# Moving the first sums of squares into the last attention pair, in an attention + gated MLP + routed experts kernel

## The chip, the cores and the metric

The kernel runs on one core of one Trainium2 chip. The metric is device time in microseconds (us) of one execution. Engines: PE is TensorE, ACT is ScalarE, DVE is VectorE, POOL is GpSimd, SP issues most DMAs.

## The reference

All in float32. Three blocks follow each other.

```python
# 1: attention, B=2, H=8, S=768, D=64; the mask keeps pairs whose 6 sign bits q@proj, k@proj agree
scores = where(mask, scale * q @ k.T, -1e9)
attn = exp(scores - max); attn /= attn.sum + 1e-9
x = (attn @ v), heads side by side          # (1536, 512)
# 2: RMS norm and gated MLP, d_ff 1536
xn = x / sqrt(mean(x * x) + 1e-6) * rms_g
y = (silu(xn @ w_gate) * (xn @ w_val)) @ w_out
# 3: one of 8 experts for each token, by argmax of y @ router
out = gate * sigmoid(...) * (relu(y @ w1[e]) @ w2[e])
```

## The kernel before

Each fp32 product is made of rounded "high" parts and remainders ("low" parts), in three matmuls (high x high, high x low, low x high), so that each operand needs a high pass (on ACT) and a low pass (on DVE or POOL).

**Attention** works on 8 pairs of heads, P = 0 to 7, the last with batch 1. One pair has 12 steps j (two heads, six tiles of 128 queries). In a step every engine's `period` does one piece of each stage, in the order of its code, and the stages lag: `scores` of step j on PE (L858, L859) into `ps_s`, `maxes` on DVE (L1441), `exps` on ACT (L1191), normalizing on POOL (L693, once in three steps), then five steps later `turn` on PE (transposes, L872, into `ps_t`), `highs` on ACT (L1201, `pT_h`), `lows` on DVE (L1459, `pT_l`), and six steps later `values` on PE (L887, L889) into a value bank, `ps_o` for even groups g of three steps and `ps_p` for odd ones. When a group's values are complete ACT copies one half (`half_out`, L1206) and DVE adds the other into `xT` (`x_out`, L1465), which counts `x_done` up by one and frees the bank. In full pairs DVE does that at the end of its step, behind its `lows`, seven steps after the group's last score. `period(7, 1, ahead=False)` is the last pair; `period(8, 0, s=False, ahead=False)` is the drain: six steps without scores in which what is left of the pair is turned and multiplied.

**The RMS norm** needs the sum of x*x over 512 columns. Tokens are in four groups tg of 384 (0 and 1 are batch 0, 2 and 3 batch 1). POOL squares and adds (`add_squares`, L652, L656) into two tiles `sums` for each of groups 0 and 1 and one tile for each of groups 2 and 3. PE adds over the partitions with matmuls that stream one column of ones (`sum_squares`, L905), three for each tile, and for groups 2 and 3 three more each for `last_square`, the squares of the last pair, which ACT makes (L1212). They land in the columns of `sum_places`, all in `ps_p`. ACT takes the root (`root`, L1218, with a table load the first time), DVE inverts (`invert`, L1472), PE turns the factors (`turn_rinv`, L930), DVE copies them out (`rows_of_factors`, L1476), and SP spreads them through DRAM. Groups 0 and 1 are summed at step 1 of the drain, behind a wait for `x_done` 30; groups 2 and 3 after it.

**The gated MLP** needs the high parts of xT times the gain (`high_xn`, L1223, on ACT), and low parts: POOL for group 0 (`lows_first`, L667 and L670), DVE for the rest (`lows_xn`, L1481). In the last pair ACT makes the four high parts of batch 0, 768 columns each, at steps 1, 2, 4 and 5. In the drain PE slips in the first products of the MLP (`early_units`, `unit`, L920), by the table `EARLY`: 2, 6, 2, 2, 2 and 2 chunks of three matmuls at steps 0 to 5. After the drain it runs the gate of group 2, whose last chunk waits for the last but one of DVE's `lows_xn`, sums groups 2 and 3, and goes on with its value, the inverse, and group 3. POOL meanwhile squares batch 1 and then splits the next weights (`split_w`, L710 and L713), the second of them as soon as `x_done` is 32. From there PE runs dense MLP work for groups and filters, and later the projection, routing and experts.

Each engine runs its own program in order; semaphores named above tie them.

Of the kernel before, what the change touches and what calls it, by code (L numbers as in the profile page):

```python
# [13 lines left out]
ALU = mybir.AluOpType  # L14
# [18 lines left out]
def build(nc, q, k, v, proj, w_gate, w_val, w_out, rms_g, router, out_gate, w1, w2, out):  # L33
# [6 lines left out]
    HT = T // 2  # L40
# [37 lines left out]
    with ExitStack() as ctx:  # L78
# [179 lines left out]
        for i in range(3):  # L258
# [17 lines left out]
                 "half_ready x_done pool_passed sp_passed "  # L276
                 "consts_made gates_in filled fill_done square_step last_squared summed rms_made rinv_made rinv_turned factors_row factors_out "
                 "gained u_made xnh_made xnl_pool xnl_dve w_split wo_split gate_made value_made sig_made silu_step hs_high hs_low y_made x2_made "
# [8 lines left out]
         half_ready, x_done, pool_passed, sp_passed,  # L287
         consts_made, gates_in, filled, fill_done, square_step, last_squared, summed, rms_made, rinv_made, rinv_turned, factors_row, factors_out,
         gained, u_made, xnh_made, xnl_pool, xnl_dve, w_split, wo_split, gate_made, value_made, sig_made, silu_step, hs_high, hs_low, y_made, x2_made,
# [21 lines left out]
        def cols_of(tg):  # L311
            return slice((tg % 2) * G, (tg % 2 + 1) * G)
# [72 lines left out]
        value_banks = (ps_o, ps_p)  # L385
        sum_places = tuple(ps_p[:, HT * tg:HT * (tg + 1)] for tg in range(TG))

# [3 lines left out]
        def high_of(tg, c):  # L391

            if tg < TG // 2:
                return c + 1
            return C + c + 1 if c < C - 1 else C + c + tg - 1

        XNH_DONE = 2 * C + 1

# [411 lines left out]
        def _(pe):  # L810
# [84 lines left out]
            def sum_squares(tg):  # L895

                pe.wait_ge(square_step, squares_until[tg])
                parts = list(sums[tg])
                if tg >= TG // 2:
                    pe.wait_ge(factors_row, 1)  # L900
                    pe.wait_ge(last_squared, tg - TG // 2 + 1)
                    parts.append(last_square[tg - TG // 2])
                for t in range(HT):
                    for n, part in enumerate(parts):
                        mm = nc.tensor.matmul(sum_places[tg][:, t:t + 1], part[:, t * P128:(t + 1) * P128],  # L905
                                              ones_f[:, 0:1], start=(n == 0), stop=(n == len(parts) - 1))
                mm.then_inc(summed, 1)
# [40 lines left out]
            def period(P, par, before=True, s=True, ahead=True):  # L948
                for j in range(PAIR_STEPS):
                    if s:  # L950
                        scores(P, par, j)
                    if not s and j == 1:
                        pe.wait_ge(x_done, 4 * LAST_PAIR + 2)
                        sum_squares(0)
                        sum_squares(1)
                    if not s and j == 3:
# [7 lines left out]
                    if not s and j in EARLY:  # L964
                        some(EARLY[j], first_units)
                    if not s and j == 2:
                        turn_rinv(0)
# [192 lines left out]
        def _(act):  # L1160
# [54 lines left out]
            def root(tgs):  # L1215
                act.wait_ge(summed, tgs[-1] + 1)
                cols = slice(HT * tgs[0], HT * (tgs[-1] + 1))
                nc.scalar.activation(rms[:, cols], ps_p[:, cols], ACT.Sqrt, bias=eps[:],  # L1218
                                     scale=1.0 / DM).then_inc(rms_made, len(tgs))

            def high_xn(b, c, cols=slice(0, S)):

                nc.scalar.activation(xn[:, b, 0, c, cols], xT[:, C * b + c, cols], ACT.Copy,  # L1223
                                     scale=gain[:, c:c + 1]).then_inc(xnh_made, 1)
# [7 lines left out]
            def period(P, par, before=True, s=True, ahead=True):  # L1232
                for j in range(PAIR_STEPS):
# [6 lines left out]
                    if jj == 2 and ((j >= LAG + 1 and s) or (j < LAG + 1 and before)):  # L1240
                        half_out(Pv, g)
                    if s and not ahead and j in (1, 2, 4, 5):
                        if j == 1:
                            act.wait_ge(gates_in, 48)
                            act.wait_ge(scores_ready, PAIR_STEPS * LAST_PAIR)
                        high_xn(0, (1, 2, 4, 5).index(j))
                    if not s and j in (0, 2, 3):
                        high_xn(1, (0, 2, 3).index(j))
                    if not s and j == 1:
                        root((0, 1))  # L1250
# [161 lines left out]
        def _(dve):  # L1412
# [55 lines left out]
            def invert(tgs):  # L1468
# [3 lines left out]
                nc.vector.reciprocal(rinv[:, cols], rms[:, cols]).then_inc(rinv_made, len(tgs))  # L1472

            def rows_of_factors(b):
                dve.wait_ge(rinv_turned, b + 1)
                nc.vector.tensor_copy(rinv_rows[b][:], ps_p[0:2 * HT, P128:2 * P128]).then_inc(factors_row, 1)  # L1476
# [7 lines left out]
            def period(P, par, before=True, s=True, ahead=True):  # L1484
                for j in range(PAIR_STEPS):
# [4 lines left out]
                    if j == 0 and before:  # L1490
                        denoms(P - 1, 3)
                    if not s and j == 2:
                        invert((0, 1))
# [15 lines left out]
                    if jj == 2 and j < LAG + 1 and not s:  # L1509
                        x_out(Pv, g)  # L1510
                    if not s and j == 2:
                        rows_of_factors(0)
                    if isinstance(P, int) and P == 0 and j in (1, 2, 3, 4):
                        bits_first(1, j - 1)
# [65 lines left out]
            period(8, 0, s=False, ahead=False)  # L1580

            lows_xn(DVE_LOWS[10:12])
            invert((2, 3))
# [242 lines left out]
```

## Time and profile before

| | |
|---|---|
| time, median of 3 runs | 809.3 us (808.05 to 812.13) |
| the profiled execution's own time | 808.94 us |
| its span | 807.2 us |
| PE busy | 766.6 us, 95% of the span |
| DVE, ACT, POOL busy | 62%, 46%, 39% |
| last pair of attention, first scores to the drain's first transposes | 210.0 to 240.0 us |
| drain and first MLP products, to the second filter | 240.0 to 279.3 us |

All times inside the span are from its start. A busy share is an average over very different stages, and TensorE's busy time does not tell at which clock it ran. The chain of waits says who ended last at each moment; the timeline of one engine names, in brackets, how long it sat idle before an instruction and who released it. An fp32 matmul or transpose appears as two records.

### The profile page before, as it was taken

The page shows a single profiled execution, that of the slowest core. Times are in us where ns is not written, and L with a number is a line of the kernel's source. Part 1 is how long each engine was busy: PE and PEld are TensorE (multiplying, and loading weights), DVE is VectorE, ACT ScalarE, POOL GpSimd, SP SyncE. Part 2 cuts the span into 40 slices and gives each one's busy share as a digit, 9 for nine tenths or more (in the row PEclk, how much of TensorE's full clock was granted, in tenths as well). Part 3 has the DMA queues.
Part 4 walks back from the last instruction along what each step waited for, and adds up shares of the span by engine and source line. Part 5 has one row for each costly group of instructions (what it writes and reads, how often), then busy time and mean ns, then how long its engine had stood idle before and what let it go on. Part 6 is the DMA issues. An engine that isn't in the chain of part 4 may idle for free.

```text
span 807.2 us, 14150 instructions
## 1 busy us (share of the span) xinstructions
PE 766.6 (95%) x4212; PEld 677.9 (84%) x4212; DVE 501.6 (62%) x979; ACT 374.7 (46%) x668; POOL 317.8 (39%) x340
## 2 busy tenths in 40 slices
PE   4899999999999999999999999999769999999996
PEld 3799888988878999999999988888548887888784
DVE  7999999999984553443343444363664566555641
ACT  5888888888983311111111234434423335553331
POOL 7877777788886363234422002211200111010110
PEclk9999999999997999999999999999979999999999
DMA  6888769656300321111210030040543365555410
GB/s 197 230 239 223 199 171 271 185 146 149 83 2 27 92 70 61 40 39 39 65 52 0 3 153 27 27 139 29 186 157 131 136 240 204 181 196 196 141 50 22
DMA packets 53716, 96.82 MB, mean 120 GB/s; under 512 B 6841, under 2 KB 21189, under 8 KB 53656
## 3 DMA queue, kind: packets, MB, share of 16 engines
q1 hardware_dynamic: 48648, 84.90, 35.5%
q10 hardware_dynamic: 2768, 4.87, 2.4%
q0 software_dynamic: 2240, 6.31, 2.0%
q8 instruction: 31, 0.51, 0.3%
q14 instruction: 29, 0.24, 0.1%
HBM read 58.51 MB, written 21.04 MB: 99 GB/s over the span
## 4 chain that ended last, share of the span: by engine, by line
PE 83%; DVE 9%; issue 3%; POOL 2%; ACT 2%; DMA 1%; ACTq 0%; POOLq 0%; DVEq 0%
PE ps_t L1046 13%; PE ps_s L920 12%; PE ps_s L1093 11%; PE ps_t L1113 11%; PE ps_t L920 6%; PE ps_t L872 6%; DVE pT_l L1459 3%; PE ps_o L920 3%; PE ps_p L920 3%; PE ps_s L859 2%; PE ps_s L858 2%; DVE negmax L1441 2%; PE ps_s L1104 2%; PE ps_o L887 1%; PE ps_o L889 1%
## 5 line engine op out<-in xcount | busy, mean ns | idle before, releaser
L693 POOL TENSOR_SCALAR probs<-probs,rden,alone 128x768 f32<-128x768 f32 x96 | 94.5, 997 | 35.2 <-DVE rden L1453 34.9
L1459 DVE TENSOR_TENSOR pT_l<-ps_t,pT_h 128x384 fp32r<-128x384 f32 x192 | 97.7, 549 | 16.1 <-ACT pT_h L1201 15.1
L801 POOL DMA_INDIRECT out_dram<-rows_out,rows_in x16 | 23.1, 1441 | 194.7 <-ACT rows_out L1356 185.2
L920 PE MATMUL ps_s<-xn,w_h 128*128 128x384 f32 x384 | 98.8, 338 | 0.2 <-POOL w_l L713 0.2
L1201 ACT ACTIVATE pT_h<-ps_t 128x384 fp32r<-128x384 f32 x192 | 85.5, 491 | 25.5 <-PE ps_t L872 24.3
L1191 ACT ACTIVATE probs<-ps_s,negmax 128x768 f32<-128x768 f32 x96 | 87.0, 907 | 19.1 <-DVE negmax L1441 18.5
L872 PE MATMUL ps_t<-ident,probs 128*128 128x128 f32 x576 | 88.4, 283 | 5.6 <-DVE pT_l L1459 2.6
L1441 DVE TENSOR_REDUCE negmax<-ps_s 128x1 f32<-128x770 f32 x96 | 90.9, 947 | 1.6 <-PE ps_s L859 1.0
L1619 DVE TENSOR_TENSOR expert_w<-piece,expert_w 128x2048 f32 (+1 forms) x32 | 72.1, 2288 | 31.8 <-ACT expert_w L1324 26.2
L1093 PE MATMUL ps_s<-expert_w,rowsT_h 128*128 (+1 forms) x256 | 83.2, 407 | 3.6 <-issue 1.8
L872 PEld LDWEIGHTS ps_t<-ident,probs 128*128 128x128 f32 x576 | 63.5, 141 | 25.6 <-DVE pT_l L1459 10.3
L1113 PE MATMUL ps_t<-expert_w,hidT_h 128*128 (+1 forms) x256 | 81.8, 400 | 1.7 <-DVE hidT_l L1774 1.4
L793 POOL DMA_INDIRECT routed<-x,dest x12 | 21.1, 1757 | 128.4 <-DVE x L1697 128.4
L920 PEld LDWEIGHTS ps_s<-xn,w_h 128*128 128x128 f32 x384 | 70.5, 191 | 0.5 <-POOL w_l L713 0.5
L1324 ACT ACTIVATE expert_w<-piece 128x2048 f32 (+1 forms) x32 | 59.6, 1907 | 17.2 <-issue 17.2
L858 PE MATMUL ps_s<-k_a,q_a 128*128 128x384 f32 x192 | 65.7, 342 | 1.8 <-ACT probs L1191 1.1
L1348 ACT ACTIVATE hidT_h<-ps_s 128x512 fp32r<-128x512 f32 x32 | 19.0, 594 | 102.7 <-PE ps_s L1104 77.1
L859 PE MATMUL ps_s<-k_b,q_b 128*128 128x384 f32 x192 | 65.6, 341 | 0.0
L920 PE MATMUL ps_s<-xn,w_l 128*128 128x384 f32 x192 | 64.7, 337 | 0.0
L1093 PEld LDWEIGHTS ps_s<-expert_w,rowsT_h 128*128 128x128 f32 x256 | 47.8, 192 | 15.2 <-issue 2.6
L1046 PE MATMUL ps_t<-wo_h,hs_h 128*128 128x512 f32 x144 | 59.3, 412 | 0.0
L1113 PEld LDWEIGHTS ps_t<-expert_w,hidT_h 128*128 128x128 f32 x256 | 46.7, 188 | 12.7 <-issue 2.7
(244 smaller groups left out, 1697.5 us busy)
## 6 DMA issues: line engine op xcount, KB each, us to landing
piece<-in_moe_w_dram SPq DMA_DIRECT2D x32, 1024.0 KB, 5.5
routed<-filler SPq DMA_DIRECT2D x52, 257.0 KB, 4.6
k_a<-qk_h SPq DMA_DIRECT2D x28, 192.0 KB
rows_in<-routed ACTq DMA_DIRECT2D x17, 257.0 KB, 2.6
rawv<-in_v_dram SPq DMA_DIRECT2D x8, 384.0 KB, 6.1
w_raw<-in_moe_w_gate_dram SPq DMA_DIRECT2D x12, 256.0 KB, 3.0
w_raw<-in_moe_w_val_dram SPq DMA_DIRECT2D x12, 256.0 KB, 3.4
wo_raw<-in_moe_w_out_dram SPq DMA_DIRECT2D x12, 256.0 KB, 2.7
```

The costliest lines, as they stand in the source:

```text
L693: nc.gpsimd.tensor_scalar(pr, pr, rden[:, j:j + 1], alone[:, j:j + 1], ALU.mult, ALU.add).then_inc(norm_done, 1)
L858: nc.tensor.matmul(o, q_a[par][:, r, queries], k_a[par][:, r, keys], start=True, stop=False)
L859: mm = nc.tensor.matmul(o, q_b[par][:, r, queries], k_b[par][:, r, keys], start=False, stop=True)
L872: mm = nc.tensor.transpose(ps_t[kt % 2][:, i * P128:(i + 1) * P128], probs[:, 3 * g + i, kt * P128:(kt + 1) * P128], ident[:])
L920: mm = nc.tensor.matmul(unit_banks[tg][w][:, 0:G], a_[par][:, w, c, :], xn_at(tg, part, c), start=(n == 0), stop=(n == 3 * C - 1))
L1046: mm = nc.tensor.matmul(ps_t[par][:], a_[par][:, f, :], b_[:, f, :], start=(f == 0 and n == 0), stop=(f == NF - 1 and n == 2))
L1093: mm = nc.tensor.matmul(ps_s[0][:, half, :], a_[:, c, :], b_[:, e_side, c, cols], start=(n == 0), stop=(n == 3 * C - 1))
L1113: mm = nc.tensor.matmul(ps_t[1][:], a_[n % 2][:, c, :], b_[:, e_side, c, :], start=(c == 0 and t == 0), stop=(c == CF - 1 and t == 2))
L1191: nc.scalar.activation(probs[:, j].rearrange("p (a n) -> p a n", a=2), third(ps_s[j % 2]), ACT.Exp, bias=negmax[:, j:j + 1], accum_out=psu ...
L1201: nc.scalar.activation(pT_h[u % 4][:], ps_t[kt % 2][:, 0:G], ACT.Copy).then_inc(high_ready, 1)
L1441: nc.vector.tensor_reduce(negmax[:, c], with_floor(ps_s[j % 2]), AX.XY, ALU.max, negate=True).then_inc(max_done, 1)
L1459: nc.vector.tensor_tensor(pT_l[u % 4][:], ps_t[kt % 2][:, 0:G], pT_h[u % 4][:].bitcast(F32), ALU.subtract).then_inc(low_ready, 1)
```

## The change

1. **High parts.** The four 768-column `high_xn` of batch 0 at steps 1, 2, 4 and 5 of the last pair become eight of 384 columns, group 0 and then group 1, at steps 1, 2, 4, 5, 7, 8, 10 and 11. `high_of` and `XNH_DONE` count accordingly.
2. **First sums.** `sum_squares(0)` and `sum_squares(1)` leave step 1 of the drain for steps 7 and 10 of the last pair, between `scores` and `turn`, in whichever value bank is between two groups (`ps_p`, then `ps_o`); each waits for `x_done` 28 and 29, that is, for that bank to be free. DVE copies three columns of sums out to `rms` each time (`sums_to_rms`), and PE waits for that before the bank is used again. `root`, `invert`, `turn_rinv` and `rows_of_factors` of batch 0 move one step forward in the drain; `root` reads `rms`.
3. **Last squares.** DVE adds `last_square` to `sums` for groups 2 and 3 (`add_last`): for group 2 in step 4 of the drain ahead of the last `x_out`, for group 3 after the drain, ahead of the last two `lows_xn`. PE then needs three matmuls instead of six for each group.

```diff
-        sum_places = tuple(ps_p[:, HT * tg:HT * (tg + 1)] for tg in range(TG))
+        sum_places = tuple((ps_p, ps_o, ps_p, ps_p)[tg][:, HT * tg:HT * (tg + 1)] for tg in range(TG))
...
         def high_of(tg, c):
+
+            if tg < TG // 2:
+                return C * tg + c + 1
+            return 2 * C + c + (1 if c < C - 1 else tg - 1)
...
-        XNH_DONE = 2 * C + 1
+        XNH_DONE = 3 * C + 1
@@ tensor, sum_squares
-                    pe.wait_ge(last_squared, tg - TG // 2 + 1)
-                    parts.append(last_square[tg - TG // 2])
+                    pe.wait_ge(last_added, tg - TG // 2 + 1)
@@ tensor, period
-                    if not s and j == 1:
-                        pe.wait_ge(x_done, 4 * LAST_PAIR + 2)
-                        sum_squares(0)
-                        sum_squares(1)
+                    if s and not ahead and j in (7, 10):
+                        pe.wait_ge(x_done, 4 * LAST_PAIR + (j - 7) // 3)
+                        sum_squares((j - 7) // 3)
+                    if s and not ahead and j == 9:
+                        pe.wait_ge(sums_out, 1)
+                    if not s and j == 0:
+                        pe.wait_ge(sums_out, 2)
...
-                    if not s and j == 2:
+                    if not s and j == 1:
+                        pe.wait_ge(x_done, 4 * LAST_PAIR + 2)
                         turn_rinv(0)
@@ scalar, period
-                    if s and not ahead and j in (1, 2, 4, 5):
+                    if s and not ahead and j % 3:
...
-                        high_xn(0, (1, 2, 4, 5).index(j))
+                        tg, c = divmod(2 * (j // 3) + j % 3 - 1, C)
+                        high_xn(0, c, cols_of(tg))
...
-                    if not s and j == 1:
+                    if not s and j == 0:
                         root((0, 1))
@@ vector
+            def sums_to_rms(tg):
+                dve.wait_ge(summed, tg + 1)
+                nc.vector.tensor_copy(rms[:, HT * tg:HT * (tg + 1)], sum_places[tg]).then_inc(sums_out, 1)
+
+            def add_last(half):
+                dve.wait_ge(last_squared, half + 1)
+                dve.wait_ge(square_step, (17, 22)[half])
+                part = sums[TG // 2 + half][0]
+                nc.vector.tensor_tensor(part[:], part[:], last_square[half][:], ALU.add).then_inc(last_added, 1)
@@ vector, period
-                    if not s and j == 2:
+                    if not s and j == 1:
                         invert((0, 1))
...
+                    if s and not ahead and j in (7, 10):
+                        sums_to_rms((j - 7) // 3)
-                    if not s and j == 2:
+                    if not s and j == 1:
                         rows_of_factors(0)
+                    if not s and j == 4:
+                        add_last(0)
@@ vector, behind the drain
+            add_last(1)
             lows_xn(DVE_LOWS[10:12])
```

On PE, at step 7 of the last pair, the order before was this (scores, then the transposes, then the values of group 0):

```order
L858 MATMUL ps_s<-k_a_114,q_a_116 128x384
L859 MATMUL ps_s<-k_b_115,q_b_117 128x384
L858 MATMUL ps_s<-k_a_114,q_a_116 128x384
L859 MATMUL ps_s<-k_b_115,q_b_117 128x384
L872 MATMUL ps_t<-ident,probs 128x128 x6
L887 MATMUL ps_o<-pT_h_128,v_hl_123 128x384
```

and is now this:

```order
L862 MATMUL ps_s<-k_a_114,q_a_116 128x384
L863 MATMUL ps_s<-k_b_115,q_b_117 128x384
L908 MATMUL ps_p<-ones_f,sums_0_166 128x1
L908 MATMUL ps_p<-ones_f,sums_1_167 128x1
L908 MATMUL ps_p<-ones_f,sums_0_166 128x1
L908 MATMUL ps_p<-ones_f,sums_1_167 128x1
L908 MATMUL ps_p<-ones_f,sums_0_166 128x1
L908 MATMUL ps_p<-ones_f,sums_1_167 128x1
L876 MATMUL ps_t<-ident,probs 128x128 x6
```

The six one-column matmuls, with their wait for the bank, stand ahead of the transposes of the same step; step 10 reads alike with `ps_o`.

On DVE, from step 4 of the drain to the inverse of batch 1, the order before was:

```order
L1459 TENSOR_TENSOR pT_l_132<-ps_t,pT_h_128 128x384
L1459 TENSOR_TENSOR pT_l_133<-ps_t,pT_h_129 128x384
L1481 SCALAR_TENSOR_TENSOR xn<-xT,gain,xn 128x384 x2
L1465 TENSOR_TENSOR xT<-ps_p,o_half 64x384
L1481 SCALAR_TENSOR_TENSOR xn<-xT,gain,xn 128x384 x2
L1472 RECIPROCAL rinv<-rms 128x6
```

and is now:

```order
L1472 TENSOR_TENSOR pT_l_132<-ps_t,pT_h_128 128x384
L1472 TENSOR_TENSOR pT_l_133<-ps_t,pT_h_129 128x384
L1504 SCALAR_TENSOR_TENSOR xn<-xT,gain,xn 128x384 x2
L1495 TENSOR_TENSOR sums_171<-sums_171,last_square_173 128x384
L1478 TENSOR_TENSOR xT<-ps_p,o_half 64x384
L1495 TENSOR_TENSOR sums_172<-sums_172,last_square_174 128x384
L1504 SCALAR_TENSOR_TENSOR xn<-xT,gain,xn 128x384 x2
L1485 RECIPROCAL rinv<-rms 128x6
```

One addition now stands ahead of the last `x_out` and one, with its wait for the last squares, ahead of the last two low parts.

## Rows read from the trace of the kernel before

**Rows 1.** The page: busy time of the engines over the whole span.

```profile
PE 766.6 (95%) x4212; PEld 677.9 (84%) x4212; DVE 501.6 (62%) x979; ACT 374.7 (46%) x668; POOL 317.8 (39%) x340
```

**Rows 2.** Timeline of PE, last pair: start us, us, engine line op out<-in count [idle before].

```profile
214.21 0.33 PE L858 MATMUL ps_s<-k_a,q_a 128*128 128x384 f32 x1
...
222.20 0.33 PE L858 MATMUL ps_s<-k_a,q_a 128*128 128x384 f32 x1
...
227.58 0.34 PE L859 MATMUL ps_s<-k_b,q_b 128*128 128x384 f32 x1
228.76 1.01 PE L872 MATMUL ps_t<-ident,probs 128*128 128x128 f32 x6 [0.84 <-DVE pT_l L1459]
...
230.31 0.33 PE L858 MATMUL ps_s<-k_a,q_a 128*128 128x384 f32 x1
...
237.13 0.33 PE L858 MATMUL ps_s<-k_a,q_a 128*128 128x384 f32 x1
```

**Rows 3.** Timeline of ACT, last pair and drain.

```profile
226.66 0.94 ACT L1223 ACTIVATE xn<-xT,gain 128x768 fp32r<-128x768 f32 x1
...
264.14 0.52 ACT L1212 ACTIVATE last_square<-xT 128x384 f32<-128x384 f32 x1
...
267.41 0.51 ACT L1212 ACTIVATE last_square<-xT 128x384 f32<-128x384 f32 x1
```

**Rows 4.** Timeline of DVE, last pair.

```profile
229.20 0.55 DVE L1465 TENSOR_TENSOR xT<-ps_p,o_half 64x384 f32<-64x384 f32 x1
...
230.77 1.02 DVE L1459 TENSOR_TENSOR pT_l<-ps_t,pT_h 128x384 fp32r<-128x384 f32 x2
...
236.02 0.55 DVE L1465 TENSOR_TENSOR xT<-ps_o,o_half 64x384 f32<-64x384 f32 x1
```

**Rows 5.** Timeline of PE, drain and behind it.

```profile
239.96 1.01 PE L872 MATMUL ps_t<-ident,probs 128*128 128x128 f32 x6
...
244.79 4.90 PE L905 MATMUL ps_p<-ones_f,sums 128*128 128x1 f32 x24 [1.62 <-DVE xT L1465]
249.55 1.52 PE L872 MATMUL ps_t<-ident,probs 128*128 128x128 f32 x6
...
259.89 0.88 PE L872 MATMUL ps_t<-ident,probs 128*128 128x128 f32 x6 [0.37 <-DVE rinv_rows L1476]
...
268.71 0.28 PE L905 MATMUL ps_p<-ones_f,sums 128*128 128x1 f32 x2
...
271.30 0.59 PE L920 MATMUL ps_t<-xn,w_h 128*128 128x384 f32 x2
```

**Rows 6.** PE by stretches: us, busy (count), granted clock, DMA share, GB/s.

```profile
241.83:245.24 3.41, 1.79 (x10) 1.00 0.52 154
245.24:255.48 10.24, 10.24 (x43) 0.50 0.00 0
269.13:272.54 3.41, 3.41 (x28) 1.00 0.00 0
272.54:275.96 3.42, 3.42 (x13) 0.50 0.00 1
```

**Rows 7.** Timeline of DVE, drain and behind it.

```profile
252.10 2.23 DVE L1481 SCALAR_TENSOR_TENSOR xn<-xT,gain,xn 128x384 fp32r<-128x384 f32 x2
...
261.00 1.02 DVE L1459 TENSOR_TENSOR pT_l<-ps_t,pT_h 128x384 fp32r<-128x384 f32 x2 [1.17 <-ACT pT_h L1201]
261.94 2.19 DVE L1481 SCALAR_TENSOR_TENSOR xn<-xT,gain,xn 128x384 fp32r<-128x384 f32 x4
...
266.31 0.55 DVE L1465 TENSOR_TENSOR xT<-ps_p,o_half 64x384 f32<-64x384 f32 x1 [0.18 <-ACT o_half L1206]
266.89 1.94 DVE L1481 SCALAR_TENSOR_TENSOR xn<-xT,gain,xn 128x384 fp32r<-128x384 f32 x2
```

**Rows 8.** Timeline of POOL, drain and behind it.

```profile
255.10 1.01 POOL L656 TENSOR_TENSOR sums<-sums,square 128x384 f32<-128x384 f32 x1
...
268.51 2.53 POOL L713 TENSOR_TENSOR w_l<-w_raw,w_h 128x1024 fp32r<-128x1024 f32 x1
```

More of the change, by code:

```diff
@@ L276, in build @@
                  "half_ready x_done pool_passed sp_passed "
-                 "consts_made gates_in filled fill_done square_step last_squared summed rms_made rinv_made rinv_turned factors_row factors_out "
+                 "consts_made gates_in filled fill_done square_step last_squared last_added summed sums_out rms_made rinv_made rinv_turned factors_row factors_out "
                  "gained u_made xnh_made xnl_pool xnl_dve w_split wo_split gate_made value_made sig_made silu_step hs_high hs_low y_made x2_made "
@@ L287, in build @@
          half_ready, x_done, pool_passed, sp_passed,
-         consts_made, gates_in, filled, fill_done, square_step, last_squared, summed, rms_made, rinv_made, rinv_turned, factors_row, factors_out,
+         consts_made, gates_in, filled, fill_done, square_step, last_squared, last_added, summed, sums_out, rms_made, rinv_made, rinv_turned, factors_row, factors_out,
          gained, u_made, xnh_made, xnl_pool, xnl_dve, w_split, wo_split, gate_made, value_made, sig_made, silu_step, hs_high, hs_low, y_made, x2_made,
@@ L1217, in root @@
                 cols = slice(HT * tgs[0], HT * (tgs[-1] + 1))
-                nc.scalar.activation(rms[:, cols], ps_p[:, cols], ACT.Sqrt, bias=eps[:],
+                source = rms
+                if tgs[0] == 0:
+                    act.wait_ge(sums_out, 2)
+                else:
+                    source = ps_p
+                nc.scalar.activation(rms[:, cols], source[:, cols], ACT.Sqrt, bias=eps[:],
                                      scale=1.0 / DM).then_inc(rms_made, len(tgs))
```

## The prediction

> **What bounds the kernel now.** I read the page first: TensorE is busy for 95% of the span and DVE for 62% [rows 1], so whatever shortens or lengthens PE's path shows in the end. Behind the drain PE runs dense products with no waits, so a shift at its end is carried to the last instruction. Everything that the change touches lies between 210 and 279 us, which I therefore read engine by engine.
>
> In the last pair the chain of waits runs mostly through DVE and ACT, not PE. Three steps take 7.99 us (214.21 to 222.20) and 8.11 us (222.20 to 230.31) where ACT makes two 768-column high parts in them, and 6.82 us (230.31 to 237.13) where it makes none [rows 2]. PE idled 0.84 us before one set of transposes [rows 2].
>
> In the drain PE idles 1.62 us for an x_out, then spends 4.76 us (244.79 to 249.55) on 24 records of one-column sums [rows 5]. The same 24 records take 2.59 us (268.71 to 271.30) later [rows 5]. The stretches tell why: the granted clock is 1.00 until 245.24 and 0.50, TensorE's 1.2 GHz level, for the next 10.24 us. Ahead of the fall PE was busy for 1.79 of 3.41 us. A second low stretch, 3.42 us, follows the second sums, although PE was busy throughout, mostly with one-column work [rows 6].
>
> **The change, step by step** (+ is slower). Sums are against the profiled execution, 808.94 us (span 807.2), 0.36 under the median of 809.3.
>
> A. *Eight high parts for four.* A 768-column part takes 0.94 us, and a 384-column piece on ACT 0.52 (the square is the nearest row) [rows 3]. Groups of three steps with two parts averaged 8.05 us. With ACT last, two pieces save 2 x 0.42 = 0.84, giving 7.21. Two groups gain 0.84 each. The last two, now with pieces as well, go from 6.82 to at most 7.21, +0.4 each: -1.7 + 0.8 = **-0.9** (ends -1.7, if the stalls of B cover the late pieces, and 0, if DVE is as late as ACT).
>
> B. *Sums inside the pair.* `x_done` 28 is counted by the x_out at 229.20 to 229.75 [rows 4], but PE has finished the scores of step 7 at 227.92 [rows 2], so it now waits almost 2 us, less what A brings DVE forward, for a free bank. Behind that come 12 records at 2.59/24 = 0.108 us, 1.3 us, and only then the transposes. From transposes to the first low part the trace has 1.11 us (259.89 to 261.00) [rows 5, 7]. With X the end of the x_out, low parts of step 7 can start at X + 0.04 + 1.30 + 1.11 = X + 2.45. In the trace they start at 230.77, X + 1.02 [rows 4]. DVE loses 1.4, and the copy of three columns takes some 0.2: 1.6. Queued behind PE's wait are the transposes, hence ACT's high parts, the next exp, and DVE's low parts. Step 10 repeats it with the x_out at 236.02 [rows 4], which again is the last thing that DVE does in the step ahead. Twice: **+3.2** (ends +1.8, if later steps take some back, and +4.6, twice the 2.3 us by which the transposes at 228.76 are put off to X + 1.34 = 231.1).
>
> C. *Front of the drain.* The idle 1.62, the sums at their full-clock price 2.6 and the 0.37 for the factors [rows 5] go: **-4.6**. Next late would be ACT, where the table load and root now stand ahead of the high parts of step 1. They fall under the x_out and low parts that DVE does there anyway, and six chunks of PE's own products cover the inverse. If that cover fails, up to 1 us: ends -5.0 and -3.6.
>
> D1. *POOL beside DVE.* Its squares end at 256.11 [rows 8], 16.1 us after the first transposes of the drain (239.96 [rows 5]), and they do not move. DVE's four low parts (261.94 [rows 7]) come 22.0 after these transposes now. Full-clock and without C's terms that is some 12. So they fall beside POOL's squares. Two such ops took 2.23 us beside POOL and four 2.19 without it [rows 7]: 1.12 against 0.55 us each. In the 4 us that are left of the squares, that is 3.5 ops x 0.57 = 2.0. DVE has a little slack there, and the first added op (0.55) stands ahead of the last x_out: **+1.5** together (ends 0 and +2.5).
>
> D2. *The second addition.* The last x_out ends at 266.86 = Y [rows 7] and the last square at 267.92 = Y + 1.06 [rows 3]. The addition must follow, then the low part that PE's last chunk ahead of the sums needs. At 0.55 to 1.12 us for each that is Y + 2.2 to Y + 3.3, where PE comes to that chunk 0.52 before 268.71 [rows 5], at Y + 1.3 or, since D1 puts Y off, Y + 0.9. **+1.9** (ends +0.9, +2.4).
>
> The Trainium skill, SBUF — State Buffer, section "SBUF: two separate sides", says that DVE (with two SBUF inputs) and GpSimd take their shared port pair as an exclusive lock for a whole instruction. Rows 7 fit it. By it the low part could wait out all of POOL's weight split, which is the third rival below.
>
> E. *Half the last sums.* 12 records fewer: **-1.3**.
>
> Sum of A to E: -0.9 + 3.2 - 4.6 + 1.5 + 1.9 - 1.3 = **-0.2 us**.
>
> F. *The clock.* What 1.2 GHz cost before: 4.76 - 2.59 = 2.2 on the sums, half of 249.55 to 255.48, 3.0, and half of 3.42, 1.7, in all 6.9 us [rows 5, 6]. These go. But the change makes three new thin places, each of 1.3 to 2 us idle with 0.6 to 1.3 us of one-column work beside it: steps 7 and 10 and the end of D2. Before, the clock fell behind an idle 1.62 us with sums after it, and again behind 2.6 us of one-column work with no idle time at all [rows 5, 6], so I expect falls after all three, one of them doubled. The shortest low stretch is 3.42 us, worth 1.7: 4 x 1.7 = 6.8. Net **-0.1** (ends -6.9 with no fall, and +6.7 with eight stretches).
>
> Forecast: 808.94 - 0.3 = 808.6 for such a run, **809.0** as a median (+0.36). Its own range is 806 to 812, by the ends of B, D2 and one stretch more or less.
>
> **The rivals.**
>
> 1. *The clock stays up in the pair.* For it: PE idled 0.84 us at full clock in the pair [rows 2]. Against: the new gaps are three times that with the sums. Only the tail falls once: F becomes -6.9 + 1.7 = -5.2, the time 809.3 - 0.2 - 5.2 = 803.9.
>
> The Trainium skill, TensorE: Matmul & The Clock Gate, section "What's actually happening", says that recent activity alone releases the throttle. By it two separate short gaps might pass where one long one did not. The fall at 245.24 fits it, but no row shows such a short gap with sums.
>
> 2. *Slower: attention does not get the clock back.* The low stretch of 10.24 us held on although PE had transposes and values from 249.55 [rows 5, 6]. If attention at 1.2 GHz is too thin to rise, all steps from 7 to the end of the pair run so. PE's work in a step is between 1.55 us (228.76 to 230.31) and 2.27 us (6.82/3) [rows 2]. Doubled that is 3.1 to 4.5, and I take 4.1. Five steps lose 1.8 each, 9 us, and the sums at step 10 another 1.3, in place of the two or three stretches counted (3.4 to 5.1): +5 to +7, the time 815. It decides if the granted clock is still 0.50 at the second scores after step 7.
>
> 3. *POOL's weight split takes the port.* It takes 2.53 us [rows 8] and starts at Y + 1.65. If the addition slips in first and the low part behind it loses, PE's chunk waits until about Y + 4.4, D2 becomes +3.5: 810.6.
>
> 4. *The waits of B bite less.* If what PE does late is made up from idle time that DVE and ACT have later in the pair, B goes to nothing: 805.8. Against: DVE's low parts follow that x_out within 1.02 us, with a maximum of its own in between [rows 4], so DVE has nothing spare there.
>
> 5. *The change does not do what it says in A:* the high parts were never last, and ACT's smaller pieces gain 0: 809.9, inside the forecast's range.
>
> **The numbers.** Chances: forecast 0.37 (rival 5 in it), first rival 0.17, second 0.16, third 0.20, fourth 0.10. A measurement of this kernel can tell about 0.5% from no change, 4.05 us: faster is below 805.25, slower above 813.35. Faster: the first rival (0.15 of it) and a share of the fourth, 0.03: 0.18. Slower: the second (0.13 of it), more stretches in the third and in the forecast, 0.06: 0.19. Within: 0.63. The range that leaves out 2 in 10 takes in the first rival's time of 803.9 and comes near the second's: 803.8 to 814.5.
>
> **What would show it.** PE waits for x_out ahead of the one-column sums at steps 7 and 10, 1.3 us or more each, and the pair, first scores to first transposes of the drain, is 2 to 5 us longer than 30.0. No sums stand in the drain, and the time from its first transposes (239.96) to those of step 3 (259.89) falls from 19.9 us to 10 to 11. PE waits behind the drain for a low part, about 2 us. The granted clock is 0.50 at about three or four places instead of two. If PE does not wait at step 7, B is wrong, and if the clock never falls in the pair, F is.

## The result, and the profile after

The change makes the kernel slower by about 2.7 us. Its median is 813.37 us (14 runs, 810.40 to 814.45) beside 810.06 for the kernel before (14 runs). The medians are 3.3 us apart; the ratio over all runs, which I go by, is 1.0033, with an interval of 1.002 to 1.0046, and makes 2.7 us. I had forecast 809.0, 0.3 below the median shown in front. The time lies inside the range and inside 0.5%, but the kernel moved, and not the way forecast.

The profiled execution took 812.65 us (span 810.8), 3.6 us more span than before. Of that 1.41 us are there before the last pair starts, where nothing was edited, and 0.54 come back behind the second filter; single executions differ by that much (over the fourteen traces of this document, whose code is the same up to there, the last pair starts at 209.8 to 211.7 us). What the edits do is the 72.03 us from the pair's first scores to the second filter, in place of 69.30: **+2.73 us**. All further tables give this stretch in pieces, read from PE's timeline: *pair* to the drain's first transposes, *front* to the transposes of its step 3, *mid* to the first record of the second sums, *end* to the second filter. Each is one execution: *front* is 19.93 us before and 18.31 in `e3_add_only` below, where nothing in it was edited, with 10.24 and 6.83 us at the low clock. So +2.73 is good to some 2 us only, and the ratios decide.

| us | pair | front | mid | end | total | stretches at granted clock 0.50 |
|---|---|---|---|---|---|---|
| before | 29.95 | 19.93 | 8.82 | 10.60 | 69.30 | 10.24 at the first sums; 3.41 |
| change | 35.75 | 10.08 | 14.71 | 11.49 | 72.03 | 3.41; 3.41; 10.24 behind the drain |

The page after, busy time of the engines:

```profile
PE 767.0 (95%) x4200; PEld 679.5 (84%) x4200; DVE 506.1 (62%) x983; ACT 375.3 (46%) x672; POOL 318.7 (39%) x340
```

Nothing in [rows 1] hints at what moved; PE's timeline does (pair, drain and behind it; columns as in [rows 2]):

```profile
229.93 1.50 PE L908 MATMUL ps_p<-ones_f,sums 128*128 128x1 f32 x12 [1.43 <-DVE xT L1478]
231.29 0.85 PE L876 MATMUL ps_t<-ident,probs 128*128 128x128 f32 x6
...
240.49 1.50 PE L908 MATMUL ps_o<-ones_f,sums 128*128 128x1 f32 x12 [1.25 <-DVE xT L1478]
241.85 0.85 PE L876 MATMUL ps_t<-ident,probs 128*128 128x128 f32 x6
...
247.17 0.92 PE L876 MATMUL ps_t<-ident,probs 128*128 128x128 f32 x6
...
257.25 0.82 PE L876 MATMUL ps_t<-ident,probs 128*128 128x128 f32 x6
...
263.93 0.44 PE L891 MATMUL ps_p<-pT_h,v_hl 128*128 128x384 f32 x1 [1.73 <-DVE pT_l L1472]
...
270.86 0.98 PE L923 MATMUL ps_t<-xn,w_h 128*128 128x384 f32 x2 [3.22 <-DVE xn L1504]
271.96 2.55 PE L908 MATMUL ps_p<-ones_f,sums 128*128 128x1 f32 x12
```

The two new waits stand where part B put them, the sums are gone from the drain, and its front takes 10.08 us (247.17 to 257.25) against 19.93 [rows 5]. Two waits are larger than I had allowed: 1.73 us at the values of step 5 of the drain and 3.22 us at the last chunk. The low clock, by stretches (columns as in [rows 6]):

```profile
228.93:232.34 3.41, 2.41 (x21) 1.00 0.00 0
232.34:235.75 3.41, 3.41 (x14) 0.50 0.00 0
239.17:242.58 3.41, 2.17 (x20) 1.00 0.00 0
242.58:245.99 3.41, 3.41 (x15) 0.50 0.00 0
266.48:269.89 3.41, 1.16 (x7) 1.00 0.33 77
269.89:280.13 10.24, 9.27 (x33) 0.50 0.00 0
```

TensorE goes to its 1.2 GHz level after each of the three places, returns after 3.41 us in attention both times, and stays there for 10.24 us behind the drain. The rest is on DVE (timeline, drain and behind it):

```profile
259.35 4.06 DVE L1504 SCALAR_TENSOR_TENSOR xn<-xT,gain,xn 128x384 fp32r<-128x384 f32 x4
...
265.90 0.55 DVE L1478 TENSOR_TENSOR xT<-ps_p,o_half 64x384 f32<-64x384 f32 x1
267.55 0.56 DVE L1495 TENSOR_TENSOR sums<-sums,last_square 128x384 f32<-128x384 f32 x1 [1.10 <-ACT last_square L1219]
268.02 3.22 DVE L1504 SCALAR_TENSOR_TENSOR xn<-xT,gain,xn 128x384 fp32r<-128x384 f32 x2
```

and on POOL:

```profile
266.54 1.05 POOL L714 TENSOR_SCALAR w_h<-w_raw 128x1024 fp32r<-128x1024 f32 x1 [4.08 <-DVE xT L1478]
267.68 2.62 POOL L717 TENSOR_TENSOR w_l<-w_raw,w_h 128x1024 fp32r<-128x1024 f32 x1
```

The four low parts that took 2.19 us take 4.06 [rows 7]. Before, the last two began right behind the x_out at 266.89, ahead of POOL's split [rows 7, 8]. Now the addition and its wait for ACT let the split begin at 267.68, and PE waits for the low part until 270.86.

### The profile page after: what moved, and what is told of

It is laid out like the page before. It is cut to its first block, busy times and chain, and to the rows that moved or that the text cites. A ratio compares the mean times of both kernels' runs of the same rounds, so it can differ in the third digit from the quotient of the medians.

```text
span 810.8 us, 14140 instructions
## 1 busy us (share of the span) xinstructions
PE 767.0 (95%) x4200; PEld 679.5 (84%) x4200; DVE 506.1 (62%) x983; ACT 375.3 (46%) x672; POOL 318.7 (39%) x340
## 4 chain that ended last, share of the span: by engine, by line
PE 81%; DVE 10%; issue 3%; ACT 2%; POOL 2%; DMA 1%; ACTq 0%; POOLq 0%; DVEq 0%
PE ps_t L1053 12%; PE ps_s L923 12%; PE ps_s L1100 11%; PE ps_t L1120 11%; PE ps_t L923 6%; PE ps_t L876 6%; DVE pT_l L1472 4%; PE ps_o L923 3%; PE ps_p L923 3%; PE ps_s L863 2%; PE ps_s L862 2%; DVE negmax L1454 2%; PE ps_s L1111 2%; PE ps_o L891 1%; PE ps_o L893 1%
```

## The experiments

Every ratio is to the kernel before on the same chip, with its 95% interval; it rests on all executions. The pieces are read from one profiled execution each, and where a low stretch fell there it need not fall in every other, so the two are kept apart below. The ratios rest on 10 or 12 executions each of `e1`, `e2`, `e5`, `e6` and `e12`, on 4 of `e11` and on 6 of each other one.

### Each part alone

`e2_pieces` is the kernel before with part 1 alone (eight pieces, new counts). `e3_add_only` is the kernel before with part 3 alone. `e1_no_add` is the change without part 3:

```diff
-                    pe.wait_ge(last_added, tg - TG // 2 + 1)
+                    pe.wait_ge(last_squared, tg - TG // 2 + 1)
+                    parts.append(last_square[tg - TG // 2])
...
-            add_last(1)
             lows_xn(DVE_LOWS[10:12])
```

(`add_last(0)` goes too.)

Expected of `e2_pieces`:

> Part 1 alone (eight high parts of 384 columns; sums and last squares as before). Theory (waits): pieces help ACT only: the three-step groups with two high parts go from 8.05 to about 7.4 us, the last two groups stay at 6.8 to 7.2, the pair is about 1 us shorter than 29.95, and the whole 0.5 to 1.5 us faster than before. Rival (ACT was never last): no change in the pair, within 0.3 us.

Expected of `e3_add_only`:

> Part 3 alone on the kernel before (DVE adds the last squares; pair and first sums as before). Port theory: the low part behind the addition starts only when POOL's 2.5 us weight split is over, PE idles about 3 us at its last chunk ahead of the second sums, the clock falls there for more than one stretch, and the whole is 2 to 5 us slower than before. Rival (only the added wait for the last squares counts): PE idles about 1 us there, the sums save 1.3 us, and the whole is within 1 us of before.

Expected of `e1_no_add`:

> The change without part 3 (PE multiplies the last squares itself again; parts 1 and 2 stay). Port theory: PE no longer idles behind the drain, one low stretch follows the second sums as in the kernel before, and the whole is 3 to 5 us faster than the change, so 0 to 2 us faster than before. Rival (the loss sits in the pair, the tail is even): as slow as the change, +2 to +3 us over before.

| us | pair | front | mid | end | total | low clock | ratio |
|---|---|---|---|---|---|---|---|
| part 1 | 29.34 | 18.63 | 8.82 | 12.21 | 69.00 | 6.83; 6.83 | 1.0000 [0.9987, 1.0012] |
| part 3 | 29.93 | 18.31 | 12.80 | 11.70 | 72.74 | 6.83; 10.24 | 1.0059 [1.0038, 1.0080] |
| parts 1, 2 | 35.70 | 10.28 | 10.71 | 10.62 | 67.31 | 6.83; 3.41 | 0.9990 [0.9970, 1.0009] |

Part 3 makes the loss: alone it costs 0.6%, and without it parts 1 and 2 come out at no change. Part 1 brings the scores of step 7 forward by 0.83 us (16.22 for 17.05 from the pair's start) and those of step 8 by 1.29, but the pair ends only 0.61 earlier, and in the whole nothing is left of it (ratio 1.0000), where 0.5 to 1.5 us were expected. Not all of the tail's loss is part 3's: without it PE still waits 1.70 us at the values of step 5 of the drain and mid is 10.71. With the shorter front of parts 1 and 2 DVE's four low parts run beside POOL's squares and take 4.04 us. What part 3 adds needs none of the other parts. `e3_add_only`, DVE's timeline behind the drain:

```profile
267.30 0.56 DVE L1477 TENSOR_TENSOR sums<-sums,last_square 128x384 f32<-128x384 f32 x1 [1.10 <-ACT last_square L1211]
267.77 3.22 DVE L1486 SCALAR_TENSOR_TENSOR xn<-xT,gain,xn 128x384 fp32r<-128x384 f32 x2
```

and PE's:

```profile
270.61 0.98 PE L919 MATMUL ps_t<-xn,w_h 128*128 128x384 f32 x2 [3.24 <-DVE xn L1486]
```

It is the change's wait to within 0.02 us.

### The sums one place later: `e5_sums_late`

In the change, the sums of steps 7 and 10 stand ahead of the transposes. Here they stand behind the step's values, DVE copies them out a step later, and PE's waits for these copies move with them:

```diff
-                        pe.wait_ge(x_done, 4 * LAST_PAIR + (j - 7) // 3)
-                        sum_squares((j - 7) // 3)
...
                         values(Pv, par if j >= LAG + 1 else 1 - par, g, jj)
+                    if s and not ahead and j in (7, 10):
+                        pe.wait_ge(x_done, 4 * LAST_PAIR + (j - 7) // 3)
+                        sum_squares((j - 7) // 3)
...
-                    if s and not ahead and j in (7, 10):
-                        sums_to_rms((j - 7) // 3)
+                    if s and not ahead and j in (8, 11):
+                        sums_to_rms((j - 8) // 3)
```

> The change with the two first sums moved behind the values of steps 7 and 10, and DVE's copies a step later. Theory (the wait for the bank is what costs): PE does not idle ahead of the sums, the pair goes from 35.75 us to 31 to 33, the clock falls in it at most once, and the whole is 3 to 5 us faster than the change. Rival (the one-column matmuls themselves cost, wherever they stand in the pair, and pull the clock down): the pair stays above 34 us with two low stretches, the whole within 1 us of the change.

Measured: pair 30.92, front 10.11, mid 14.25, end 10.87, total 66.15; ratio 0.9967 [0.9949, 0.9986]. PE in the pair:

```profile
229.15 1.02 PE L876 MATMUL ps_t<-ident,probs 128*128 128x128 f32 x6 [0.38 <-DVE pT_l L1472]
...
230.71 1.39 PE L908 MATMUL ps_p<-ones_f,sums 128*128 128x1 f32 x12
...
238.89 1.40 PE L908 MATMUL ps_o<-ones_f,sums 128*128 128x1 f32 x12
```

No wait stands ahead of the sums, the clock stays at 1.00 in the pair, and the pair is 4.8 us shorter than in the change. The place of the sums was worth more than the whole change cost (5.3 us by the ratios). In the tail this execution idles 1.75 us at the values of step 5 and 1.70 at the last chunk, and has 3.41 and 6.83 us at the low clock behind them. Against part 1 alone, the two sums cost the pair 30.92 - 29.34 = 1.6 us.

### The wait without the idle time: `e12_fill`

Is it the idle time ahead of the sums, or the sums, that brings the clock down? Twelve 128-column products run on PE ahead of each wait, into unused columns of the other bank, the one that takes this step's values (work that the kernel doesn't need; no output depends on it):

```diff
                     if s and not ahead and j in (7, 10):
+                        for _ in range(12):
+                            nc.tensor.matmul(value_banks[(j - 7) // 3][:, G:G + P128], q_a[par][:, 1, 0:P128],
+                                             k_a[par][:, 1, 0:P128], start=False, stop=False)
                         pe.wait_ge(x_done, 4 * LAST_PAIR + (j - 7) // 3)
```

> The change with twelve more 128-column matmuls ahead of PE's wait for the bank at steps 7 and 10, written to columns nobody reads: PE's idle time there is filled with dense work, the waits and all else stay. It tells the clock's share of the loss in the pair from that of the waits. If the fills keep the clock at 2.4 GHz: no low stretch in the pair, the pair goes from 35.75 to about 33 us, and the whole is 2 to 3 us faster than the change. If the one-column matmuls pull the clock down by themselves: both low stretches stay, pair and whole as in the change.

Measured: pair 34.45, front 10.03, mid 14.20, end 9.26, total 67.94; ratio 1.0003 [0.9988, 1.0018]. PE by stretches:

```profile
228.04:232.00 3.96, 3.82 (x33) 1.00 0.01 2
237.18:240.50 3.32, 3.14 (x28) 1.00 0.02 5
240.90:244.30 3.40, 3.40 (x16) 0.55 0.00 0
```

As a test of the clock it says little. With the idle time down to 0.14 and 0.18 us, the clock stays up at step 7, but at step 10, with the same fill, it falls all the same. And `e1_no_add`, whose pair is the change's, with no fill at all, stays up at step 7 too:

```profile
227.80:231.20 3.40, 2.87 (x23) 1.00 0.00 0
231.20:234.60 3.40, 3.40 (x26) 1.00 0.00 0
234.60:238.00 3.40, 1.94 (x14) 1.00 0.02 5
238.02:241.43 3.41, 3.41 (x17) 0.52 0.00 0
241.43:244.84 3.41, 3.41 (x14) 0.50 0.51 143
```

It pays with 6.83 us in one piece after step 10, and so does `e10_reorder`; the change and `e6_pool_waits` have 3.41 at either step. All four have 6.8 us at 0.50, and pairs of 35.70 to 35.90. What `e12_fill` gives is a price: with 3.41 us of it instead of 6.8 the pair is 1.30 us shorter than the change's, and 1.25 shorter than that of `e1_no_add`, whose sums of step 10 start at the same 27.67 us of the pair. I put a low stretch in attention at 1.3 us, not the 1.7 of half its length; the stretch that is left in `e12_fill` has no run to price it.

Its tail is the change's, with no edit in it, and comes out otherwise. PE waits as long for the low part, but has 3.41 us at the low clock behind it instead of 10.24, and the end takes 9.26 us for 11.49:

```profile
269.22 0.59 PE L923 MATMUL ps_t<-xn,w_h 128*128 128x384 f32 x2 [3.24 <-DVE xn L1507]
```

```profile
267.84:271.25 3.41, 2.03 (x16) 1.00 0.00 0
271.25:274.66 3.41, 3.41 (x12) 0.50 0.00 0
```

So what this wait costs through the clock differs between executions by over 2 us.

### POOL's split behind the low parts: `e6_pool_waits`

```diff
             pool.wait_ge(x_done, 4 * PAIRS)
+            pool.wait_ge(xnl_dve, len(DVE_LOWS))
             run(split_w(1, 1))
```

(and the same wait further down goes.)

> The change, but POOL starts the second weight split only when all low parts are made. Port theory: the low part behind the addition takes 0.55 us instead of waiting out the 2.6 us split, PE's idle time ahead of its last chunk falls from 3.22 to 0.5 to 1.2 us, the low stretch behind the drain shrinks from 10.24 us to 3.4 or 6.8, and the whole is 3 to 5 us faster than the change (even with before or 1 to 2 us faster). Rival (the wait for the last squares is what PE sees): PE still idles over 2 us there, the whole within 1 us of the change.

Measured: pair 35.90, front 10.03, mid 12.14, end 7.72, total 65.79; ratio 0.9989 [0.9972, 1.0005]. DVE behind the drain:

```profile
267.94 0.56 DVE L1495 TENSOR_TENSOR sums<-sums,last_square 128x384 f32<-128x384 f32 x1 [1.10 <-ACT last_square L1219]
268.42 1.14 DVE L1504 SCALAR_TENSOR_TENSOR xn<-xT,gain,xn 128x384 fp32r<-128x384 f32 x2
```

and PE:

```profile
269.18 0.59 PE L923 MATMUL ps_t<-xn,w_h 128*128 128x384 f32 x2 [1.14 <-DVE xn L1504]
269.78 1.39 PE L908 MATMUL ps_p<-ones_f,sums 128*128 128x1 f32 x12
```

The same two low parts take 1.14 us instead of 3.22 once POOL's 2.62 us instruction is out of their way, and PE's idle time falls by as much, 3.22 to 1.14. The sums behind them then run at full clock, so the end takes 7.72 us for 11.49. The split itself ends some three microseconds later and PE waits for nothing of it in these pieces. By these pieces the edit saves 6.2 us (72.03 - 65.79), by the ratios 0.44%, some 3.6. The execution of the change that was profiled had the long low stretch behind the drain, and that of `e12_fill` shows that not all have it.

### The needed low part ahead of the addition: `e10_reorder`

PE's last chunk ahead of the second sums needs group 2's last low part. The others belong to group 3, which comes later. So DVE makes group 2's first, and all four of group 3 last:

```diff
-        DVE_LOWS = ([(1, c) for c in range(C)] + [(2, c) for c in range(C - 1)] + [(3, c) for c in range(C - 1)]
-                    + [(2, C - 1), (3, C - 1)])
+        DVE_LOWS = [(tg, c) for tg in (1, 2, 3) for c in range(C)]
...
+            lows_xn(DVE_LOWS[7:8])
             add_last(1)
-            lows_xn(DVE_LOWS[10:12])
+            lows_xn(DVE_LOWS[8:12])
```

(the slices of steps 3 and 4 become [4:6] and [6:7].)

> The change, with DVE's low parts of group 3 all moved behind the second addition: two instead of four low parts at step 3 of the drain, one instead of two at step 4, and the low part that PE's last chunk needs ahead of the addition. Theory: the idle 1.73 us at the values of step 5 falls under 0.5, since two low parts fewer alternate with POOL's squares; PE no longer idles at its last chunk, but up to 1 us at the sums for the addition; the whole 3 to 5 us faster than the change. Rival: the group 3 low parts now stand beside POOL's split and are late for the gate of group 3, PE idles 2 us or more there, the whole within 1 us of the change.

Measured: pair 35.70, front 10.14, mid 8.91, end 8.84, total 63.59; ratio 0.9951 [0.9933, 0.9970]. The mid stretch is back to 8.91 us, against 8.82 in the kernel before and 14.71 in the change: both D1 and D2 are gone with one new order of DVE's twelve low parts. By the ratios that is 6.6 us off the change, more than the 3 to 5 expected. What is left is a small wait of PE, because the inverse stands behind group 3's four low parts, which now meet POOL's split:

```profile
269.14 0.27 PE L932 MATMUL ps_p<-ident,rinv 128*6 128x128 f32 x1 [0.89 <-DVE rinv L1484]
```

### All three mends, and each taken away again

`e11_all_mends` joins e5, e6 and e10. `e15_late_reorder` leaves out e6's edit, `e7_late_poolwaits` leaves out e10's, `e14_mended_no_add` has all three without part 3 (the squares are summed by PE again), and `e13_mended_four_pieces` all three without part 1. `e11` ran on another chip than these four, each beside the kernel before on its own chip.

Expected of `e11_all_mends`:

> The change with three mends together: first sums behind the values (as in the late-sums run), low parts of group 3 behind the second addition, POOL's split behind all low parts. If the losses add up as the theory has it: pair 31 us, from the drain's first transposes to those of step 3 10 us, from there to the second sums 10 to 11, low stretches one or none, the whole 6 to 9 us faster than the change, 3.5 to 6 us faster than before. Rival (what one wait gives back the next takes): not over 1 us faster than the late-sums run.

Of `e15_late_reorder`:

> All mends but POOL's second weight split starts at once, as in the change. Port theory: the second addition or a low part of group 3 waits out the 2.6 us split, PE idles 1 to 3 us at the second sums or at the gate of group 3, with a low stretch, and the whole is 1 to 5 us slower than with all mends. Rival (with the needed low part ahead of the addition the split hurts nobody): within 1 us.

Of `e7_late_poolwaits`:

> All mends but the low parts of group 3 stay where the change has them (four at step 3 of the drain, beside POOL's squares). Theory: PE idles 1.7 us at the values of step 5 and about 1.1 us at the last chunk, with one or two low stretches, and the whole is 3 to 6 us slower than with all mends. Rival (the idle times there were only fatal together with the split): within 2 us.

Of `e14_mended_no_add`:

> All mends but part 3 undone: PE multiplies the last squares itself, 24 records of one-column work in a row instead of 12, with no idle time around them. If one-column work by itself pulls the clock down: one low stretch behind the second sums, the whole 2.5 to 3.5 us slower than with all mends (1.3 for the records, 1.7 for the clock). If only idle time does: no low stretch, 0.5 to 1.3 us slower.

Of `e13_mended_four_pieces`:

> All three mends, but with the four 768-column high parts of the kernel before (part 1 undone). Theory: the part 1 run gained 0.8 us by step 7 and lost part of it to the later pieces; here the same, the pair 0.3 to 1.0 us longer than 30.9, the whole 0.3 to 1.0 us slower than with all mends. Rival (without the clock's falls the pieces are worth their full 0.8 or more): over 1 us slower.

| us | pair | front | mid | end | total | low clock | ratio |
|---|---|---|---|---|---|---|---|
| e11 | 30.91 | 10.10 | 8.92 | 7.72 | 57.65 | none | 0.9860 [0.9838, 0.9882] |
| e15 | 30.92 | 10.10 | 8.93 | 8.84 | 58.79 | none | 0.9880 [0.9851, 0.9909] |
| e7 | 30.91 | 10.12 | 12.28 | 7.72 | 61.03 | 3.41 | 0.9917 [0.9889, 0.9945] |
| e14 | 30.90 | 10.10 | 8.93 | 10.64 | 60.57 | 3.41 | 0.9892 [0.9863, 0.9921] |
| e13 | 31.59 | 9.58 | 8.88 | 7.76 | 57.81 | none | 0.9868 [0.9840, 0.9896] |

`e11_all_mends` takes 799.0 us beside 810.68: it beats both kernels by more than 11 us. By the ratios it is 14 us faster than the change, where 6 to 9 were expected. In its four pieces PE has no low clock:

```profile
211.37:242.28 30.91, 29.14 (x194) 1.00 0.04 10
242.28:252.38 10.10, 9.96 (x62) 1.00 0.19 53
252.38:261.30 8.92, 8.92 (x55) 1.00 0.24 69
261.30:269.02 7.72, 7.72 (x50) 1.00 0.14 52
```

The reordering is the larger of the two tail mends (e7 lacks it and is 3.4 us longer here); POOL's wait is worth 1.1 us once the order is right, and the ratios of e11 and e15 overlap. Part 1 is worth 0.16 us in the mended kernel, and the ratios of e11 and e13 can't be told apart.

Part 3, which made the change slower, is worth 2.92 us in these traces once mended (60.57 - 57.65), more than twice the 1.3 us of its twelve records. e14 shows why, PE by stretches around its 24 records (from 259.97 on):

```profile
258.50:261.90 3.40, 3.40 (x28) 1.00 0.21 77
262.00:262.40 0.40, 0.40 (x6) 0.88 0.00 0
262.40:265.90 3.50, 3.50 (x13) 0.53 0.00 0
```

PE is busy all the time here, mostly with one-column work, and the clock falls; with half the records, in e11, it does not. The ratios, 0.9860 and 0.9892, differ the same way, though their intervals overlap, so that the gain of part 3 is not shown beyond the traces. Two things were not run: the mended kernel without part 2, and the reordering and POOL's wait on the kernel before. The kernel before has no wait in mid (8.82 us), so I expect little of them there.

## Why the prediction was wrong

| step | forecast, us | measured, us |
|---|---|---|
| A + B, at full clock | +2.3 | +3.2 |
| the clock in the pair (F) | +3.4 | +2.6 |
| C and the clock in the front (F) | -9.8 | -9.85 |
| D1 | +1.5 | +2.2 |
| D2 | +1.9 | +3.1 |
| E and the rest to the second filter (with F) | +0.4 | +1.5 |
| sum | -0.3 | +2.7 |

The measured column adds up, to rounding, to the 2.73 us of the traces. Of the 5.80 us that the pair is longer, two low stretches at 1.30 are the clock's 2.6, an estimate with the price of `e12_fill`, and the other 3.2 are A + B. D1 is the time from the transposes of step 3 to the end of the last x_out, 9.20 us for 6.97; D2 that from there to PE's last chunk, 4.41 for 1.33.

**A** was right in mechanism and too large. I took a piece at 0.52 us from the row of the square; on ACT it takes 0.60 to 0.62 (`e2_pieces`):

```profile
222.87 0.60 ACT L1223 ACTIVATE xn<-xT,gain 128x384 fp32r<-128x384 f32 x1
```

Two pieces then save 0.65 us of the two parts at 0.93, and so it came: the three groups take 7.32, 7.47 and 7.47 us for 7.99, 8.11 and 6.82. That is 0.67 and 0.64 gained where I had 0.84 twice, and 0.65 lost where I had 0.4. The pair ends 0.61 us earlier for part 1 alone and 0.68 in the mended kernel, of which 0.16 is left at the second filter, and no ratio shows it. **B** was right in mechanism. PE waits 1.43 and 1.25 us for x_out. A + B came to 0.9 above the forecast, 0.3 of it from A and 0.6 from B. `e5_sums_late` shows that it was a matter of place. **C** and the clock given back there came out to 0.1 us, which is in part luck: they were worked out from the profiled execution of the kernel before and are compared with it, and with its front at 18.31 us, as in `e3_add_only`, they would be 1.6 less.

**D2 is the step that failed.** I put it at +1.9 by taking the low part behind the addition at 0.55 to 1.12 us, and gave POOL's split a rival of its own with a chance of 0.20. That rival came true: the two low parts behind the addition took 3.22 us, the first of them 2.69, PE waited 3.22, D2 was +3.1 a little under the rival's +3.5, and `e6_pool_waits` takes two thirds of the wait away by moving POOL alone (1.14 us for 3.22). The forecast should have held it. I left POOL's split where it was, at Y + 1.65, so that the low part, ready at Y + 1.6, might still slip in. But POOL's instruction ahead of the split had run beside the very low parts that the change moves away. It took 1.47 us in the kernel before,

```profile
266.95 1.47 POOL L710 TENSOR_SCALAR w_h<-w_raw 128x1024 fp32r<-128x1024 f32 x1 [10.84 <-DVE xT L1465]
```

and takes 1.05 in the change, 1.05 in `e3_add_only`, and again 1.47 in `e10_reorder`, where a low part stands beside it. With DVE waiting for the last square, the split began at Y + 1.23 (267.68, the x_out ending at 266.45), and the low part was ready at Y + 1.6. With D2 and what hangs on it in the tail, 1.2 and 1.1 us, comes 2.3 of the 3.0 us by which the sum is off. The rest is A + B and D1, too small by 1.6, less the clock in the pair, too large by 0.8.

The Trainium skill, SBUF — State Buffer, section "SBUF: two separate sides", has this lock for a whole instruction, and the trace agrees: two low parts need 1.14 us with POOL idle and 3.22 beside a POOL instruction of 2.62.

**D1** was too small, 2.2 for 1.5, by "a little slack there". There was none to speak of: PE waited 1.73 us at the values of step 5. The four low parts took 4.06 us for 2.19, 1.9 us more, of the 2.0 worked out.

**F** was right in the pair, 6.8 us at 0.50, though each stretch costs 1.3 and not 1.7. In the tail it was three stretches of 3.41 us instead of two, 10.24 us at 0.50 after an idle 3.22, and this is the second half of the miss: with the idle time at 1.14 (`e6_pool_waits`) there is no fall, and the end takes 7.72 us instead of 11.49. How many stretches follow is in part chance: `e3_add_only` had 10.24 us behind the same wait, `e12_fill` 3.41. Between these two executions D2's wait costs 2.6 us in mid and another 3.8 behind it, in the clock; the ratios put both together at 3.6. I had added the two as if they did not depend on each other.

**The rivals.** The first (clock stays up in the pair) fell: the pair has 6.8 us at 0.50 in each of the four traces with this code. The rule beside it, from the Trainium skill, TensorE: Matmul & The Clock Gate, section "What's actually happening", is that activity releases the throttle. The trace agrees in the pair, where the same sums have the low clock behind them with the idle time (the change) and not without it (`e5_sums_late`), but the short gaps did not pass. The second (attention does not get the clock back) fell: it was back at 1.00 after 3.41 us both times, and after 6.83 in `e1_no_add`. The third came true in its own place, though the total came out 2.8 us above its 810.6 with D1 and the tail's clock. The fourth (B bites less) fell: A + B cost 0.9 more than forecast, not less. The fifth, that A gains nothing, has the outcome right for the whole kernel and the reason wrong: ACT's high parts did come last, as the groups of 7.99 and 8.11 us that went to 7.32 and 7.47 show.

What stays open is where exactly the clock falls: the same code had its low time at steps 7 and 10 or at step 10 alone, and the same second sums were followed by 3.41 us before and by 6.83 in `e2_pieces`. An idle 1.70 to 1.75 us at the values of step 5 had a low stretch behind it in `e5_sums_late` and `e7_late_poolwaits`, and none in the change, `e1`, `e6` and `e12`. Whether filled idle time would hold the clock is not settled either.

## What to carry to other kernels

An instruction put ahead of another can cost not its own time but what it lets in between. Here a 0.55 us addition, with its wait of 1.10, let a 2.6 us instruction of the neighbour go first, the low part took 2.7 us instead of 0.6, and TensorE's clock was low for 10.24 us behind its wait in two traces and for 3.41 in a third. Ask of each inserted wait who starts in that gap. Then order what is behind it by when it is needed: the same three parts that made this kernel 0.3% slower stand in one that is 1.4% faster, with the sums behind the step's other products, the one needed low part ahead of the addition, and POOL's split behind them all.

## What the hardware did that I had not expected

- **The clock fell behind twenty-four one-column records with PE busy throughout, and not behind twelve.** In `e14_mended_no_add` 24 records with no idle time ahead have 3.41 us at 0.50 from 262.30 on; behind the second sums of the kernel before, `e1_no_add` and `e2_pieces`, 24 as well, it was 3.41, 3.41 and 6.83. Twelve such records with no idle time close ahead had no fall behind them (`e5_sums_late` in the pair, `e11_all_mends`: clock 1.00). Twelve behind an idle 1.43 or 1.25 us had, in the change. In `e1_no_add` the clock stayed up behind an idle 1.43 us and twelve records at step 7, and the pair then had the same 6.8 us in one piece at step 10.
- **While POOL works, DVE's instruction on two SBUF operands can wait out a whole instruction.** Two low parts took 1.14 us alone, 2.2 beside POOL's squares and additions of 0.8 to 1.2 us, and 3.22 beside its 2.62 us split. It goes the other way too: POOL's `w_h` took 1.47 us beside a low part and 1.05 without.
- **A short wait was free, and a longer one cost twice.** In the profiled executions, behind the drain, 1.14 us idle ahead of twelve records left the clock up (`e6_pool_waits`). Behind 3.22 and 3.24 us it was low for 10.24 (the change, `e3_add_only`), and behind 3.24 for 3.41 (`e12_fill`).
